# Outputs of the second MLP four tiles behind h2 in place of three, with four buffers of turned ln and eight places of statistics

## The reference

```
h = x @ w_in
e = np.exp(h - h_max)
sm = e / (np.sum(e, axis=-1, keepdims=True) + 1e-09)
solu = h * sm
mu = np.mean(solu, axis=-1, keepdims=True)
var = np.mean((solu - mu) ** 2, axis=-1, keepdims=True)
ln = (solu - mu) / np.sqrt(var + 1e-06) * g_ln
return (ln @ w_out).astype(np.float32)
```

## Time and profile before

| | us |
|---|---|
| median of three timed runs | 476.73 |
| lowest and highest of them | 475.34 and 477.12 |
| the profiled execution | 474.92 |
| its span, first to last instruction | 473.1 |
| TensorE busy in it | 465.4 |
| VectorE busy | 274.3 |
| ScalarE busy | 208.0 |
| GpSimd busy | 73.9 |

### The profile page before, as it was taken

One profiled execution on the slowest core, in us unless ns is written; L12 is line 12 of the kernel. 1 busy time (PEld: TensorE's weight loads), 2 busy tenths in 40 slices (PEclk: granted clock), 3 DMA queues, 4 the chain that ended last, 5 costly groups with the idle time before them and its releaser, 6 DMA issues.

```text
span 473.1 us, 7703 instructions
## 1 busy us (share of the span) xinstructions
PE 465.4 (98%) x2894; PEld 427.8 (90%) x2894; DVE 274.3 (58%) x529; ACT 208.0 (44%) x525; POOL 73.9 (16%) x72
## 2 busy tenths in 40 slices
PE   8999999999999999999999999999999999999996
PEld 6799999999999999999999999999888888888874
DVE  5988787985444444644443244444757777666640
ACT  3986666553434334533334233333433344433331
POOL 2320000330000000000000000000034355333330
PEclk9999999999999999999999999999999999999998
DMA  8999533222300110321100321211235523532231
GB/s 303 297 359 359 160 86 94 64 93 81 125 30 30 31 58 30 115 78 30 30 1 1 89 90 46 89 46 64 72 89 116 129 67 70 118 81 67 67 68 67
DMA packets 52453, 46.01 MB, mean 97 GB/s; under 512 B 27552, under 2 KB 41792, under 8 KB 52416
## 3 DMA queue, kind: packets, MB, share of 16 engines
q1 hardware_dynamic: 52416, 45.52, 32.6%
HBM read 32.77 MB, written 6.29 MB: 83 GB/s over the span
## 4 chain that ended last, share of the span: by engine, by line
PE 86%; issue 7%; DVE 3%; DMA 2%; ACT 1%; POOL 1%; SPq 0%; DVEq 0%; POOLq 0%; ACTq 0%
PE bank L939 26%; PE bank L967 26%; PE bank L1065 14%; PE bank L1083 11%; PE bank L861 4%; PE bank L916 3%; PE bank L886 2%; DMA turned_planes<-planes 1%; DMA q_first<-q_head 1%; POOL planes L451 1%; PE bank L895 1%; PE bank L867 1%; ACT probs L467 1%; DVE neg_max L651 0%; DVE probs L647 0%
## 5 line engine op out<-in xcount | busy, mean ns | idle before, releaser
L939 PE MATMUL bank<-x_hi,win_hi 128*128 128x384 f32 x256 | 87.8, 343 | 0.0
L678 DVE TENSOR_TENSOR sqr<-relu 128x384 f32<-128x384 f32 x64 | 35.7, 557 | 88.0 <-ACT relu L516 87.7
L967 PE MATMUL bank<-h_hi,wout_hi 128*128 128x384 f32 x256 | 85.9, 335 | 0.0
L939 PE MATMUL bank<-x_hi,win_lo 128*128 128x384 f32 x256 | 85.7, 335 | 0.0
L967 PE MATMUL bank<-h_hi,wout_lo 128*128 128x384 f32 x256 | 85.6, 335 | 0.0
L939 PE MATMUL bank<-x_lo,win_hi 128*128 128x384 f32 x256 | 85.6, 334 | 0.0
L967 PE MATMUL bank<-h_lo,wout_hi 128*128 128x384 f32 x256 | 85.5, 334 | 0.0
L516 ACT ACTIVATE relu<-bank 128x384 f32<-128x384 f32 x64 | 31.5, 492 | 108.2 <-PE bank L939 107.9
L451 POOL COPY planes<-cen 128x2048 uint16<-128x2048 uint16 x12 | 33.6, 2801 | 197.1 <-DVE cen L820 197.1
L939 PEld LDWEIGHTS bank<-x_hi,win_hi 128*128 128x128 f32 x256 | 48.1, 188 | 0.5 <-DVE win_lo L687 0.3
L939 PEld LDWEIGHTS bank<-x_lo,win_hi 128*128 128x128 f32 x256 | 48.2, 188 | 0.0
(11 more groups left out here) (78 smaller groups left out, 726.4 us busy)
## 6 DMA issues: line engine op xcount, KB each, us to landing
q_sb<-qT SPq DMA_DIRECT2D x24, 192.0 KB, 2.7
win_raw<-w_in_t SPq DMA_DIRECT2D x8, 512.0 KB, 11.6
wout_raw<-w_out_t SPq DMA_DIRECT2D x8, 512.0 KB, 12.4
win_raw<-w_t SPq DMA_DIRECT2D x8, 512.0 KB, 3.4
v_ext<-vwin SPq DMA_DIRECT2D x24, 144.0 KB, 2.9
k_raw<-kT SPq DMA_DIRECT2D x8, 400.0 KB, 4.2
out<-o_sb SPq DMA_DIRECT2D x12, 256.0 KB, 3.0
v_first<-vrows SPq DMA_DIRECT2D x4, 384.0 KB, 7.9
```

Of the source, the lines that this page charges most:

```text
L678: nc.vector.tensor_tensor(sqr[:, n % 3, :], relu[:, n % 2, :], relu[:, n % 2, :], ALU.mult)\
L939: last = nc.tensor.matmul(up_bank(n), win[a][:, f * WC + k * P:f * WC + (k + 1) * P], x[b][:, c % 2, k * CH:(k + 1) * CH], start=(k == 0 a ...
L967: last = nc.tensor.matmul(down_bank(d), wout[a][:, f * WC + d * P:f * WC + (d + 1) * P], h[b][:, n % 3, :], start=(f == 0 and a == 0 and b ...
```

## The change

TensorE's, ACT's and SP's loops become one step longer, and the output, o_sb and store of a tile come four steps behind its h2 in place of three. Turned ln (lnT_hi, lnT_lo) has four buffers in place of two, and lies where the high part of the first MLP's w_out lay; the statistics have eight places in place of four. The waits are adapted: lnT_hi of tile s - 1 waits for the output of tile s - 5, and a place of statistics for o_sb eight tiles before. The rest of the memory keeps its addresses (a filler stands where lnT_hi was).

```diff
+        parts = ExitStack()
+        lnT_hi = sb(parts, "lnT_hi", [P, 4, FF2], F32R)
+        lnT_lo = sb(parts, "lnT_lo", [P, 4, FF2], F32R)
+        parts.close()
         wout_hi = sb(ctx, "wout_hi", [P, F1 * WC], F32R)
...
-        lnT_hi = sb(ctx, "lnT_hi", [P, 2, FF2], F32R)
         o_sb = sb(ctx, "o_sb", [P, 2, DM], F32)
+        sb(ctx, "hid_rest", [P, 8 * CH - 2 * DM], F32)
...
-        lnT_lo = sb(mlp2, "lnT_lo", [P, 2, FF2], F32R)
-        stat = sb(mlp2, "stat", [P, 4, 16], F32)
+        stat = sb(mlp2, "stat", [P, 8, 16], F32)
...
-            for i in range(TT + 3):
+            for i in range(TT + 4):
                 if i + 2 < (NCHUNK - 2) * TPC:
                     sp.wait_ge(h2_ok, i + 1)
                     load_y(i + 2)
                 if i < TT:
                     turn(i)
-                if i >= 3:
-                    store(i - 3)
+                if i >= 4:
+                    store(i - 4)
...
-                if i >= 4:
-                    pool.wait_ge(o_ok, i - 3)
+                if i >= 8:
+                    pool.wait_ge(o_ok, i - 7)
...
-            for s in range(TT + 3):
-                p, w = s % 2, s % 4
+            for s in range(TT + 4):
+                p, w = s % 2, s % 8
...
-                    if s >= 3:
-                        act.wait_ge(o_ps, s - 2)
-                    nc.scalar.copy(lnT_hi[:, 1 - p, :], lnT[:, 1 - p, :]).then_inc(lnhi_ok, 1)
-                if s >= 3:
-                    act.wait_ge(rstd_ok, s - 2)
-                    act.wait_ge(o_ps, s - 2)
                     if s >= 5:
-                        act.wait_ge(o_out[1 - p], 16 * ((s - 3) // 2))
-                    nc.scalar.activation(o_sb[:, 1 - p, :], bank[:, 5 - p, :], ACT.Copy,
-                                         scale=stat[:, (s - 3) % 4, 8:9]).then_inc(o_ok, 1)
+                        act.wait_ge(o_ps, s - 4)
+                    nc.scalar.copy(lnT_hi[:, (s - 1) % 4, :], lnT[:, 1 - p, :]).then_inc(lnhi_ok, 1)
+                if s >= 4:
+                    act.wait_ge(rstd_ok, s - 3)
+                    act.wait_ge(o_ps, s - 3)
+                    if s >= 6:
+                        act.wait_ge(o_out[p], 16 * ((s - 4) // 2))
+                    nc.scalar.activation(o_sb[:, p, :], bank[:, 4 + p, :], ACT.Copy,
+                                         scale=stat[:, (s - 4) % 8, 8:9]).then_inc(o_ok, 1)
...
-                    if s >= 4:
-                        dve.wait_ge(o_ok, s - 3)
+                    if s >= 8:
+                        dve.wait_ge(o_ok, s - 7)
...
-            for s in range(TT + 3):
+            for s in range(TT + 4):
...
-                if s >= 3:
-                    o = s - 3
+                if s >= 4:
+                    o = s - 4
...
-                            last = nc.tensor.matmul(bank[:, 4 + o % 2, :], ln[a][:, o % 2, f * P:(f + 1) * P],
+                            last = nc.tensor.matmul(bank[:, 4 + o % 2, :], ln[a][:, o % 4, f * P:(f + 1) * P],
```

More of the change, by code:

```diff
@@ L453, in _ @@
                   .then_inc(split_ok, 1)
-                if i >= 4:
-                    pool.wait_ge(o_ok, i - 3)
+                if i >= 8:
+                    pool.wait_ge(o_ok, i - 7)
                 pool.wait_ge(vare_ok, i + 1)
-                nc.gpsimd.tensor_tensor(stat[:, i % 4, 8:9], stat[:, i % 4, 7:8], minus_half[:, :], ALU.pow)\
+                nc.gpsimd.tensor_tensor(stat[:, i % 8, 8:9], stat[:, i % 8, 7:8], minus_half[:, :], ALU.pow)\
                   .then_inc(rstd_ok, 1)
@@ L837, in _ @@
                     dve.wait_ge(lnhi_ok, s)
-                    nc.vector.tensor_tensor(lnT_lo[:, 1 - p, :], lnT[:, 1 - p, :], lnT_hi[:, 1 - p, :].bitcast(F32),
-                                            ALU.subtract).then_inc(lnlo_ok, 1)
+                    nc.vector.tensor_tensor(lnT_lo[:, (s - 1) % 4, :], lnT[:, 1 - p, :],
+                                            lnT_hi[:, (s - 1) % 4, :].bitcast(F32), ALU.subtract).then_inc(lnlo_ok, 1)
         @block.tensor
```

## The result

The changed kernel takes 478.1 us in the median against 475.0 for the kernel before; the ratio is 1.0066, with a 95% interval of 1.0047 to 1.0084. That is 3.1 us more (2.2 to 4.0). A repeat on another occasion gave 1.0082 (1.0052 to 1.0111). The forecast was slower by 3.4.

The account below looks back on a forecast made before the run. TensorE, busy 98%, was taken as the bound. Old end -3.7, wait for y +4.1, clock +1.7, wait before output 10 +1.3 gave +3.4 us, so 479.8 us; range 477.4 to 482.6.

Parts of the forecast that it names:

- The wait for y of tile 4, 4.1: Middle, between h2 of tiles 3 and 4: TensorE waits 4.1 us for a load issued behind turn(1).
- The clock behind it, 1.7: Middle, after the wait for y of tile 4: TensorE's clock falls, 1.7 us more, bounds 0 to 3.5.
- T at 444.6: T is the end of h2 of tile 11, the last: 444.28 us before, 444.6 forecast after the change.
- DVE and ACT: Between the middle and T: DVE's steps hold TensorE up by 0; ACT's loosened waits cost nothing.
- tile 5: Middle, h2 of tile 5: its y lands at 371.9 us, in time, so no further wait.
- The wait of 1.3 before output 10: End: output 10 waits 1.3 us for o_sb of tile 8, behind lnT_hi of tile 11; lower bound 0.
- Rival 2: Middle stall and clock fall, but no wait at the end, as the transposing DMA lands in 4.3: +2.1 us; chance 0.17.
- The old end, 3.7: Kernel before, output 11: 2.0 us waiting for tile 11's data plus 1.7 of slower clock, both removed by the change.
- the 0.5% that it set as its bound: Whole kernel: the smallest effect a measurement can tell from no change, about 0.5%, 2.4 us.
- its base: Time of the kernel before that the effect is added to: median of three runs 476.73, mean of four times 476.0.

Follow-up runs that it names:

- the two kernels shown: The changed kernel with only tile 4's load of y earlier, 1.0014 to the kernel before; the changed kernel with output 0 ahead of h2 of tile 4, 1.0017.

## Why the prediction was right, point by point

- **The wait for y of tile 4, 4.1.** Right: 4.07 and 4.13 in the two profiles, landing 3.4 and 3.5 behind the issue. The earlier load alone took the whole price away.
- **The clock behind it, 1.7.** Right: counted as the prediction does, 1.7 and 1.5 in the two profiles, and in all 20 executions of the changed kernel the mean clock was 0.996 or less.
- **T at 444.6.** From the end of tile 3's h2 that is 444.6 - 357.2 = 87.4; measured 446.67 - 359.28 = 87.4. DVE and ACT cost nothing on the way, nor did tile 5, as forecast.
- **The wait of 1.3 before output 10.** Not there: 0. The term was taken from the landing of 5.8, though eleven rows spoke for 4.3. That the late landing was a meeting with an instruction load, which in the new order starts 8.3 and 10.3 after that DMA's issue in the two profiles, was in none of my rows. Rival 2 was what the profiles show: of the 4.1 between the two profiled spans 2.0 arise before the end of tile 3's h2, and the 2.1 behind it are rival 2's sum.
- **The old end, 3.7.** Its mechanism was right, its size was that of one execution. Over many it is 2.0 of waiting and 1.7 in at most 45 of 81, or some 2.9.

The last two were off by 1.3 and 0.8 in opposite directions. With the measured terms the sum is -2.9 + 5.7 = +2.8 (5.8 and 5.6 in the two profiles), where 3.1 (2.2 to 4.0) was measured. So +3.4 came that near in part by luck: without the wait that wasn't there the prediction's own terms give +2.1, which is less than the 0.5% that it set as its bound. The time of 479.8 is 1.7 above the 478.1 measured: 1.4 of it because its base, between the median of three and the mean of four, was 476.4, where the median of sixteen is 475.0, and 0.3 by the effect.

What beats both kernels: four behind with the early loads, 472.0 (0.992). The old order with moved code is at 0.994, with intervals that overlap; but it keeps 0.3 to 0.5 of waiting and no room, while four behind has some 3.6 us (21.8 against 18.2, even with a late landing) between tile 11's data and the need for them. Output 10 has only 0.3 of room for o_sb of tile 8 in that order, and 4.5 with o_sb ahead of lnT_hi (it ends at T + 11.7, and is needed at T + 16.1). The early loads have little room too: y of tile 4 lands 1.5 and y of tile 5 1.3 ahead of need.

## What to carry to other kernels

Before moving a block of the busiest engine forward, look up each semaphore that the block waits for and when its producer is issued. Here 1.5 us of room were enough in the old order, and the new one asked for 5.4. A load that stands behind a wait in its queue has to be moved with the block that needs it. And take the size of a loss at the end from several executions: the one profile had the clock's fall, and 36 of 81 other executions had none.

## What the runs showed of the hardware

**An instruction load can hold up the last packets of a DMA.** Where one on the queue q8 started 3.7 to 4.0 us after the issue of the transposing DMA (six cases), that DMA landed in 5.8 to 6.0; with none between issue and landing in 4.2 to 4.4 (133 cases). A smaller one on the queue q14 that started 3.8 after did nothing (two cases, both landed in 4.3). Moving TensorE's code by some 50 instructions took the late landing away and 2.8 us (1.8 to 3.8) of the kernel's time. That the last packet decides fits what the Trainium skill says in "DMA: Bandwidth & Descriptors", section "Why a DMA increments its semaphore by 16 and not by 1": the engines of a DMA finish independently, and only the full count says that all has landed. The load of tile 5's y in the kernel before, 5.0 where others took 3.4, had an instruction load beside it too (near 370, 3.0 after its issue). But a load 2.8 to 3.1 after the issue left it at 3.3 to 3.6 in other places (12 loads of tile 2, and tile 5 in the run with the new buffers alone). How the engines share between the two isn't shown.

**The same wait brings the clock down in one execution and not in the next.** With 2.0 of waiting the mean clock was 0.996 or less in 45 of 81, a few of them perhaps by a fall at the start; with 2.3 to 2.5 in 14 of 20, but not in the profiles of the two kernels shown (5.72 for the block behind, mean clock 1.000); with 4.1 in 20 of 20; and with no wait over 0.5 in the second MLP in 6 of 54. The Trainium skill says in "TensorE: Matmul & The Clock Gate", Part 1, of the slow matmuls at a kernel's start that their count varies between runs of one kernel. What varies here is whether the clock falls at all, late in a kernel; no run here counts the matmuls at the start. In these runs falls were more frequent with longer waits, and the fall cost 1.5 to 1.7.
